# A gate's logits computed with the tokens as the stationary operand, in place of four packed column strips and a second matmul

## The reference

```python
# x: the 2304 tokens of 512 features after the dense layer
skip_score = x @ w_skip
do_compute = skip_score > 0
xc = x[do_compute]
logits = xc @ w_gate                       # 8 experts
e_idx = np.argmax(logits, axis=1)
probs = softmax(logits)                    # in full in the reference
gate_w = probs[np.arange(len(xc)), e_idx]
for e in range(E):
    mask = e_idx == e
    h = np.maximum(xc[mask] @ w1[e], 0.0)
    y[mask] = gate_w[mask, None] * (h @ w2[e])
out[do_compute] = xc + y
```

## Time and profile before

| | |
|---|---|
| time, median of 3 runs | 718.58 us (717.32 to 718.74) |
| profiled execution | 718.74 us |
| its span | 717.1 us |
| mean granted clock of TensorE | 0.991 |
| PE busy | 671.2 us, 94% |
| PE weight loads busy | 576.4 us, 80% |
| DVE busy | 392.6 us, 55% |
| ACT busy | 369.4 us, 52% |
| POOL busy | 159.3 us, 22% |

### The profile page before, as it was taken

The page is one execution under the profiler, slowest core; times in us unless marked ns, Lnnn a source line. Parts: engine busy times, 40 slices in busy tenths (PEclk is TensorE's granted clock), DMA queues, the critical chain, the costliest instruction groups (busy, mean ns, idle before and its releaser), DMA issues.

```text
span 717.1 us, 14298 instructions
## 1 busy us (share of the span) xinstructions
PE 671.2 (94%) x4533; PEld 576.4 (80%) x4534; DVE 392.6 (55%) x1363; ACT 369.4 (52%) x1043; POOL 159.3 (22%) x211
## 2 busy tenths in 40 slices
PE   3889999999999999999999999999978899999990
PEld 3678888888888889889898988998857688887870
DVE  4867764555456434253343433445575876577664
ACT  4778766555656333333333333344436865457661
POOL 5345312231223002010010000100222433303431
PEclk9999999999999999999999999999999999999996
DMA  7547634223321331102001020023118886557761
GB/s 254 190 131 251 208 121 162 73 73 132 102 73 40 119 121 30 60 1 89 1 19 70 0 88 0 0 74 89 46 46 260 281 259 212 188 179 240 243 210 40
DMA packets 48215, 85.60 MB, mean 119 GB/s; under 512 B 7618, under 2 KB 11714, under 8 KB 48160
## 3 DMA queue, kind: packets, MB, share of 16 engines
q1 hardware_dynamic: 43664, 79.20, 33.6%
q0 software_dynamic: 3952, 4.65, 2.2%
q10 hardware_dynamic: 544, 1.05, 0.4%
HBM read 70.84 MB, written 18.52 MB: 125 GB/s over the span
## 4 chain that ended last, share of the span: by engine, by line
PE 81%; issue 5%; DVE 4%; POOL 4%; ACT 2%; DMA 2%; POOLq 1%; DVEq 0%; SPq 0%; ACTq 0%
PE ph L1345 27%; PE px L1358 27%; PE pe_h L1445 8%; PE py L1471 7%; PE pscore L1295 3%; PE ptrans L1304 2%; PE pctx L1317 2%; DMA w_raw<-we 1%; PE ph L1369 1%; PE phT L1457 1%; POOL probs L651 1%; DMA xg<-x_dram,gather_slots 1%; DVE w_lo L952 1%; ACT w_hi L772 1%; PE pxT L1425 1%
## 5 line engine op out<-in xcount | busy, mean ns | idle before, releaser
L1345 PE MATMUL ph<-x_hi,w_hi 128*128 128x256 f32 x576 | 166.2, 289 | 0.8 <-DVE x_lo L1013 0.8
L1108 DVE SCALAR_TENSOR_TENSOR gated<-gated,ph 128x256 f32<-128x256 f32 x144 | 60.5, 420 | 188.1 <-ACT gated L849 188.0
L1345 PE MATMUL ph<-x_lo,w_hi 128*128 128x256 f32 x576 | 160.6, 279 | 0.0
L1345 PE MATMUL ph<-x_hi,w_lo 128*128 128x256 f32 x576 | 160.4, 279 | 0.0
L1358 PE MATMUL px<-w_hi,g_hi 128*128 128x512 f32 x288 | 117.7, 409 | 0.0
L1345 PEld LDWEIGHTS ph<-x_hi,w_hi 128*128 128x128 f32 x576 | 108.5, 188 | 7.9 <-issue 3.3
L1358 PE MATMUL px<-w_hi,g_lo 128*128 128x512 f32 x288 | 113.6, 394 | 0.0
L1358 PE MATMUL px<-w_lo,g_hi 128*128 128x512 f32 x288 | 113.0, 392 | 0.0
L1345 PEld LDWEIGHTS ph<-x_lo,w_hi 128*128 128x128 f32 x576 | 108.9, 189 | 3.6
L1345 PEld LDWEIGHTS ph<-x_hi,w_lo 128*128 128x128 f32 x576 | 108.8, 189 | 0.0
L849 ACT ACTIVATE gated<-ph 128x256 f32<-128x256 f32 x144 | 54.9, 381 | 102.3 <-PE ph L1345 102.3
(11 more groups left out here) (201 smaller groups left out, 1101.9 us busy)
## 6 DMA issues: line engine op xcount, KB each, us to landing
w_raw<-we SPq DMA_DIRECT2D x72, 256.0 KB, 3.2
more_raw<-we SPq DMA_DIRECT2D x72, 256.0 KB, 4.0
w_raw<-wf SPq DMA_DIRECT2D x32, 256.0 KB, 3.9
vs<-vw SPq DMA_DIRECT2D x16, 384.0 KB, 3.4
qs<-qT SPq DMA_DIRECT2D x16, 288.0 KB, 3.8
ks<-kT SPq DMA_DIRECT2D x16, 288.0 KB, 4.2
xT_dram<-x_stage SPq DMA_DIRECT2D x16, 288.0 KB, 3.1
x_lo<-xT_dram SPq DMA_DIRECT2D x8, 512.0 KB, 3.8
```

Source lines behind the costliest of these rows:

```text
L1108: nc.vector.scalar_tensor_tensor(gated[s % 2][:, :], gated[s % 2][:, :], 1.0, ph[s % 2][:, 0:TT], ALU.add, ALU.mult).then_inc(gated_done, 1)
L1345: last = nc.tensor.matmul(ph[f % 2][:, 0:TT], up_w(w, k, f), x[p][:, k, :], start=(at == 0 and n == 0), stop=(at == KD - 1 and n == 2))
```

## The change

The gate's matmuls change sides: for each block of 128 tokens, four matmuls with `x2T[:, j, k]` (128x128) stationary and `gate_w[:, k]` moving add up in PSUM to the logits of that block, tokens on partitions. `gate_parts`, `copy_parts`, `logit_parts`, `same_column` and two semaphores go. `GW`, the number of columns of `gate_w`, becomes 96. The logits are made at step 6 and the ranks at step 9. In the last tile both blocks stand before the groups of `e_up`, and three groups stand between logits and ranks.

```diff
-GW = 32
+GW = 96
-PART_STEP, LOGIT_STEP, RANK_STEP = 6, 7, 10
+LOGIT_STEP, RANK_STEP = 6, 9
...
         def plogit_in(bank):
-            return bank[:, TT:TT + TJ * (E + 1)].rearrange("p (j e) -> p j e", e=E + 1)
+            return bank[:, TT:TT + TJ * GW].rearrange("p (j e) -> p j e", e=GW)
...
-            link(nc.gpsimd.memset(same_column[:, :], 0.0))
-            for k in range(KD):
-                link(nc.gpsimd.affine_select(out=same_column[:, :], in_=same_column[:, :], compare_op=ALU.not_equal, fill=1.0,
-                                             base=-GW * k, pattern=[[-1, E + 1]], channel_multiplier=1))
...
             def copy_x2T(t, i, bank):
-                wait(act, logit_parts_done, t)
+                wait(act, logits_done, t)
-            def copy_parts(t, bank):
-                act.wait_ge(logit_parts_done, t + 1)
-                wait(act, logits_done, t)
-                nc.scalar.activation(logit_parts[:, :], pparts_in(bank), ACT.Copy).then_inc(logit_parts_copied, 1)
...
-                nc.vector.tensor_copy(logits[:, :, :], plogit_in(bank)).then_inc(logits_copied, 1)
+                nc.vector.tensor_copy(logits[:, :, :], plogit_in(bank)[:, :, 0:E + 1]).then_inc(logits_copied, 1)
...
-            def gate_parts(bank):
+            def gate_block(j, bank):
                 for k in range(KD):
-                    last = nc.tensor.matmul(pparts_in(bank)[k * GW:(k + 1) * GW, :], gate_w[:, k, :],
-                                            x2T[:, :, k, :], start=True, stop=True)
-                last.then_inc(logit_parts_done, 1)
+                    last = nc.tensor.matmul(plogit_in(bank)[:, j, :], x2T[:, j, k, :], gate_w[:, k, :],
+                                            start=(k == 0), stop=(k == KD - 1))
+                return last
             def gate_logits(t, bank):
-                pe.wait_ge(logit_parts_copied, t + 1)
+                pe.wait_ge(x2T_copied, (t + 1) * 2 * TJ)
                 for j in range(TJ):
-                    last = nc.tensor.matmul(plogit_in(bank)[:, j, :], logit_parts[:, j * P:(j + 1) * P], same_column[:, :],
-                                            start=True, stop=True)
+                    last = gate_block(j, bank)
                 last.then_inc(logits_done, 1)
...
             pe.wait_ge(x2T_copied, (NT - 1) * 2 * TJ + TJ)
+            gate_block(0, px2[1])
             pe.wait_ge(last_x2T_copied, 1)
-            gate_parts(px2[1])
-            e_up(0, 0, 0, 1, range(1))
-            gate_logits(NT - 1, px2[1])
-            e_up(0, 0, 0, 1, range(1, KD - 1))
+            gate_block(1, px2[1]).then_inc(logits_done, 1)
+            e_up(0, 0, 0, 1, range(KD - 1))
             gate_ranks(NT - 1, px2[1])
```

More of the change, by code:

```diff
@@ L64 @@
 LV = 3
-GW = 32
+GW = 96
 RW = (TJ + 1) * E
-assert KD * GW == P and E + 1 <= GW
 assert NB == FB and DM == CH and NB % SLOTS == 0
@@ L201, in program @@
         gate_w = sb("gate_w", [P, KD, GW])
-        same_column = sb("same_column", [P, E + 1])
         slot_base = sb("slot_base", [P, E])
@@ L252, in program @@
         x2T = sb("x2T", [P, TJ, KD, P], to=ffn)
-        logit_parts = sb("logit_parts", [P, TT], to=ffn)
         logits = sb("logits", [P, TJ, E + 1], to=ffn)
@@ L275, in px2T_in @@
             return bank[:, TT:TT + 2 * P].rearrange("p (k t) -> p k t", t=P)
-        def pparts_in(bank):
-            return bank[:, TT:2 * TT]
         def plogit_in(bank):
-            return bank[:, TT:TT + TJ * (E + 1)].rearrange("p (j e) -> p j e", e=E + 1)
+            return bank[:, TT:TT + TJ * GW].rearrange("p (j e) -> p j e", e=GW)
         def prank_in(bank):
@@ L354, in program @@
         last_x2T_copied = sem("last_x2T_copied")
-        logit_parts_done = sem("logit_parts_done")
-        logit_parts_copied = sem("logit_parts_copied")
         logits_done = sem("logits_done")
@@ L845, in tile @@
                         copy_x2T(t - 1, T_STEPS[s], ph[s % 2])
-                    if not is_first(t) and s == PART_STEP:
-                        copy_parts(t - 1, ph[s % 2])
                     wait(act, g_lo_done, t * FB + s - 1)
@@ L902, in _ @@
             relu(0, 0, 0)
-            copy_parts(NT - 1, px2[1])
             expert_hi(0, 0, EARLY_CH + 1)
@@ L1402, in tile @@
                         transpose_x2(t - 1, T_STEPS[s], ph[s % 2])
-                    if not is_first(t) and s == PART_STEP:
+                    if not is_first(t) and s == LOGIT_STEP:
                         if isinstance(t, int) and t == 1:
                             pe.wait_ge(gate_w_in, 16)
-                        pe.wait_ge(x2T_copied, t * 2 * TJ)
-                        gate_parts(ph[s % 2])
-                    if not is_first(t) and s == LOGIT_STEP:
                         gate_logits(t - 1, ph[s % 2])
```

## The result

The changed kernel took 728.1 us (median of 6 runs, 726.68 to 730.04) against 718.66 us before (6 runs on the same chip, 717.32 to 720.0): ratio 1.0142, 95% interval 1.0117 to 1.0167. It is slower by 9.4 us, where 4.2 was forecast, and outside the range. Its profiled execution took 726.63 us for a span of 725.0; the mean granted clock is 0.991, as before.

A forecast was written before the change was run, and what follows sets the result against it. TensorE was taken to bound the kernel, busy 81% of the span. Gate +4.4, start -0.4 and last gate +0.2 summed to +4.2 us, 722.8 us from the 718.58 median; range 720.6 to 725.6.

The forecast's parts named there:

- The gate on PE after: New gate on TensorE in each loop tile: 16 instructions at 0.11 us, 1.76 less the old 1.21, +0.55 us a tile.
- The choice of 0.11 us an instruction: Pace of the new gate's instructions, set by the weight load as in `idle`'s two loads; 0.086 if only the stream counted.
- The rival with loads 0.2 apart: Gate's weight loads not hidden: 0.196 us a pair, +1.93 us a tile, 735.2 us in all; chance 5%.
- The last gate: Last tile's gate before the routed experts: its last instruction ends at 523.16, moving all behind it by +0.2 us.
- The start: GpSimd's opening work without `same_column`: first `probs` 1.32 us earlier, but only 0.4 us comes through, so -0.4 us.
- What else moves in a tile: Other shifts in loop tiles, logits, ranks and `scatter_slots` a step earlier: taken as 0, up to 0.3 us x 3.
- PE's next `ph` steps unchanged: Sign of being right: a tile alone is 0.55 us longer, with TensorE's `ph` steps after the gate unchanged.
- The third rival: The order costs more: late DVE, `idle`, late `h_hi`, slower instructions, no start gain; up to 2.6 us over, 725.4; chance 10%.

The follow-up runs named there:

- the restored place: The changed kernel with an unused 64-byte tensor behind `gate_w`, so later tensors stand 1024 bytes above their old place: 719.88 us, ratio 1.0028.

## Why the prediction was wrong

By its own steps:

- **The gate on PE after, +0.55 us a tile: right.** At the restored place a loop tile is 47.18 us for 46.59, +0.59, 4.7 us for 8 tiles for the forecast 4.4. The choice of 0.11 us an instruction from the `idle` pair over 0.086 held, and 32 columns in place of 96 changed nothing (what the streams cost is hidden). The rival with loads 0.2 apart is refuted.
- **The last gate, +0.2: its length right, its worth not.** 2.19 us for 1.92, +0.27. But the prediction let both forms start at the same release, 521.07. The old form's first load stood idle for 0.36 us before it, and the new one's does not: from the last `px` group to `top` it is 7.17 us for 7.27, -0.1 (7.17 with the 64 bytes too; 7.21 to 7.35 in the other traces of the old gate).
- **The start, -0.4: wrong size.** The first two norms came at 10.73 and 12.30 (forecast 10.7 and 12.37), so the step on GpSimd was right. The first `ph` was 1.78 us earlier: the norms' gain, 0.3 to 0.9 with the clock held, and TensorE's clock, which rose earlier in this execution. The prediction did not look at the score matmuls' 1.60 us near 37 as half clock.
- **"What else moves in a tile: I take 0": wrong.** It named `scatter_slots` as moved, and asked only whether VectorE would be late. It did not ask what stood behind the scatters on GpSimd before, where the trace already showed TensorE idle for 1.00 us at 154.99. Taking them from ahead of that norm is worth -1.68 us.
- **"PE's next `ph` steps unchanged": wrong, and it decides the case.** The sum had no term for the memory plan. The diff shows `GW` from 32 to 96 and two tensors gone; that the 1728 `ph` matmuls then stream `x` from another place was not weighed at all, as a term or as a rival. It cost 6.6 us by the last `px` group (first start at 523.55 for 516.93, the changed kernel with and without the 64 bytes; both start tile 0 within 0.01 us of each other) and 8.2 us in the medians.

Now the sum closes. To the last `px` group, in the profiled executions: -1.74 start (at the first `px`), +4.7 gate, -1.68 scatters, +6.6 place, together +7.9; measured +7.83. The third rival named a dearer order and no place that a trace then showed. Without the move the change would have cost 1.2 us, with the median under the forecast's lower end too: gains were missed as well as the loss. Part of the start's gain is the clock in these two executions and not the change; with 0.3 to 0.9 us for the start, the terms give 2.0 to 2.6 us for the change without the move, which the interval of 0.4 to 3.7 holds as well.

What stays open is the mechanism of the distance. That the place of `x` against the weights sets most of the pace of `ph` is shown: it is slow at remainders by 512 of 128, 256 and 320 and fast at 192 with `g` at 192 too, wherever the whole stands. Why 192 is good for `ph`, and 448 and 0 for the experts' matmuls, and how the place of `g` reaches `ph`, is not shown. The Trainium skill, "SBUF — State Buffer", Operand start alignment, asks only that an operand start at a multiple of its element size, and says that this is about legality, not speed; all placements here satisfy it, and they differ by up to 8 us.

## What to carry to other kernels

A change that alters the size of any on-chip tensor moves all that is allocated behind it. Compare the memory plans of the two programs, and where the other operands of the matmuls have moved against the weights, pad the plan back, here by 64 bytes, before judging the change. Where a matmul-bound kernel is tuned, try a few paddings of the operands against the weights first. When work moves in an in-order queue, look at what it stood ahead of: the wait that vanishes is in the old trace already.

## What the runs showed of the hardware

- In plain steps, TensorE never idle, the second six `ph` matmuls (fp32r, 256 columns) came 114 or 120 ns apart, the experts' (512 columns) 229 or 233, by where the operands lie in SBUF against each other; 64 bytes suffice, 512 bytes change nothing, and moving both operands together changes nothing. The first six `ph` of a step were 120 to 123 ns apart in every kernel.
- Moving by 64 bytes `g` and what is allocated behind it, which other engines use and these matmuls do not read, took `ph` from 114 to between 117 and 118 ns.
- A plain f32 matmul on a fresh 128-column block costs 0.11 us an instruction, whether 32 or 96 columns are streamed.
- The packed 128x32 loads started 0.36 us behind the end of the load before them, in the loop and in the last gate; full 128x128 loads in their place started 0.04 us behind it in the last gate.
- With the same instructions up to 40 us, the time at which TensorE's clock rose moved the first dense matmul by 0.9 to 1.2 us between executions.
